# Who splits the first head's keys and queries, and how many idle transposes stand ahead of the first scores

## The reference

```python
q_bucket = sum((q @ proj > 0) * 2**arange(6));  k_bucket likewise
scores = where(q_bucket == k_bucket, q @ k.T / 8, -1e9)
attn = softmax(scores) @ v                       # x = heads side by side
x = sigmoid(causal_conv5(x, conv_w)) * (x @ w_val) @ w_out
xk, xr = mixes of x and the token before it (mu_k, mu_r)
out = sigmoid(xr @ w_r) * (relu(xk @ w_k)**2 @ w_v)
```

## Time and profile before

| | |
|---|---|
| median of 3 runs | 484.13 us (483.76 to 484.45) |
| the profiled execution | 483.76 us, span 482.0 us |
| TensorE matmuls busy | 471.7 us (98% of the span) |
| VectorE, ScalarE, GpSimd busy | 345.4, 279.0, 260.0 us |

### The profile page before, as it was taken

How to read it: one execution, slowest core, us unless ns; L and a number is a source line. 1 busy time by engine, 2 the same in 40 slices (tenths; PEclk the granted TensorE clock), 3 DMA queues, 4 the chain that set the end, 5 groups by cost and what they waited for, 6 DMA issues and landing times.

```text
span 482.0 us, 9492 instructions
## 1 busy us (share of the span) xinstructions
PE 471.7 (98%) x3541; PEld 400.3 (83%) x3541; DVE 345.4 (72%) x607; ACT 279.0 (58%) x597; POOL 260.0 (54%) x258
## 2 busy tenths in 40 slices
PE   7899999999999999999999999999999999999997
PEld 6766767666676776777779999999999999999997
DVE  5887897988888888887747977876668569326211
ACT  4977878878787987876745451442443353344230
POOL 5795647374472745652197683575455457346140
PEclk9999999999999999999999999999999999999999
DMA  6210310404021030200220001001000000100101
GB/s 231 67 55 18 106 48 4 136 17 137 16 62 78 18 136 18 71 19 18 88 87 1 3 1 45 0 1 46 2 1 29 17 2 1 45 1 1 45 1 44
DMA packets 10557, 20.69 MB, mean 43 GB/s; under 512 B 1680, under 2 KB 6928, under 8 KB 10512
## 3 DMA queue, kind: packets, MB, share of 16 engines
q1 hardware_dynamic: 10224, 19.94, 12.6%
q10 hardware_dynamic: 288, 0.15, 0.1%
HBM read 16.94 MB, written 3.15 MB: 42 GB/s over the span
## 4 chain that ended last, share of the span: by engine, by line
PE 74%; DVE 13%; issue 6%; ACT 3%; POOL 2%; DMA 2%; SPq 0%; DVEq 0%; ACTq 0%; POOLq 0%
PE ps L732 24%; PE ps L720 14%; PE ps L740 11%; PE ps L696 10%; PE ps L685 10%; DVE tmp_b L1011 2%; DVE gate L920 2%; ACT probs L497 2%; PE ps L706 2%; DVE tmp_b L986 1%; DVE tmp_a L988 1%; DVE negmax L877 1%; DVE pt L884 1%; PE ps L668 1%; DVE x L910 1%
## 5 line engine op out<-in xcount | busy, mean ns | idle before, releaser
L877 DVE TENSOR_REDUCE negmax<-ps 128x1 f32<-128x768 f32 x96 | 91.7, 956 | 23.6 <-PE ps L685 22.9
L685 PE MATMUL ps<-k,q 128*128 128x384 f32 x384 | 92.2, 362 | 3.4 <-ACT probs L497 2.8
L497 ACT ACTIVATE probs<-ps,negmax 128x768 f32<-128x768 f32 x96 | 86.5, 901 | 10.4 <-DVE negmax L877 10.0
L696 PE MATMUL ps<-ident,probs 128*128 128x128 f32 x576 | 82.3, 275 | 1.2
L696 PEld LDWEIGHTS ps<-ident,probs 128*128 128x128 f32 x576 | 66.8, 140 | 11.9 <-DVE pt L884 4.7
L685 PEld LDWEIGHTS ps<-k,q 128*128 128x128 f32 x384 | 62.8, 189 | 15.4 <-ACT probs L497 10.6
L720 PE MATMUL ps<-pt,vals 128*64 128x384 f32 x384 | 68.8, 494 | 0.0
L447 POOL TENSOR_TENSOR h_lo<-tmp_b,h_hi 128x256 fp32r<-128x256 f32 x48 | 39.3, 824 | 45.2 <-ACT h_hi L599 45.2
L505 ACT ACTIVATE pt<-ps 128x384 f32<-128x384 f32 x96 | 46.9, 488 | 18.8 <-PE ps L696 15.0
L732 PE MATMUL ps<-xk_hi,w_hi 128*128 128x256 f32 x192 | 53.9, 281 | 0.3 <-POOL xk_lo L441 0.3
L884 DVE COPY pt<-ps 128x384 f32<-128x384 f32 x96 | 52.1, 542 | 2.8 <-PE ps L696 2.8
(11 more groups left out here) (86 smaller groups left out, 1107.0 us busy)
## 6 DMA issues: line engine op xcount, KB each, us to landing
w_raw<-w SPq DMA_DIRECT2D x8, 640.0 KB, 6.1
raw_q<-qT SPq DMA_DIRECT2D x8, 384.0 KB, 4.5
raw_k<-kT SPq DMA_DIRECT2D x8, 384.0 KB, 3.4
vals<-v SPq DMA_DIRECT2D x16, 192.0 KB, 2.4
out<-w_raw SPq DMA_DIRECT2D x24, 128.0 KB, 1.7
w_raw<-w SPq DMA_DIRECT2D x4, 512.0 KB, 3.3
codes_b<-codes ACTq DMA_DIRECT2D x1, 128.0 KB, 4.3
proj_bd<-proj ACTq DMA_DIRECT2D x1, 16.0 KB, 3.4
```

Of the source, the lines that this page charges most:

```text
L497: act.activation(probs[par][:, :], score[par], ACT.Exp, bias=negmax[:, t:t + 1], accum_out=sums[:, t, 0:1]).then_inc(exp_done, 1)
L685: last = pe.matmul(ps[:, 2 * par + half, 0:HALF], qq[h][:, q], kk[h][:, half * HALF:(half + 1) * HALF], start=first, stop=not first)
L696: last = pe.transpose(tbank[u][:, k * P:(k + 1) * P], probs[g % 2][:, kt * P:(kt + 1) * P], ident[:, :])
L877: dve.tensor_reduce(negmax[:, t:t + 1], score[g % 2], AX.XY, ALU.max, negate=True).then_inc(max_done, 1)
```

## The change

GpSimd no longer makes the low keys of head 0: it starts with the low queries of head 0, then low keys and low queries of head 1. VectorE makes the low keys of head 0, in a new function `first_low_keys`, after the first of its two casts of head 0's high keys and ahead of `bits_out(0)`; the second cast of head 0 moves behind `bits_out(0)`. `high_keys` on VectorE now makes one half at a time, and the wait for the keys' load stands once ahead of the first. TensorE has 10 idle transposes ahead of `scores(0)` instead of 14.

```diff
--- before.py
+++ after.py
@@ -364,9 +364,9 @@
                                base=0, pattern=[[-1, P]], channel_multiplier=1).then_inc(ident_up, 1)
 
             pool.wait_ge(ident_up, 1)
-            for head in range(2):
-                low_keys(head)
-                low_queries(head)
+            low_queries(0)
+            low_keys(1)
+            low_queries(1)
             pool.wait_ge(qlo_done, 2)
 
             for i in range(PAIRS):
@@ -757,7 +757,7 @@
             pe.wait_ge(codes_in, 16)
             for j in range(4):
                 match(0, j)
-            keep_busy(14)
+            keep_busy(10)
             scores(0)
             scores(1)
             for g in range(PAIRS * TILES):
@@ -883,12 +883,12 @@
                 dve.wait_ge(tr_done[1], g + 1)
                 dve.tensor_copy(pt[head % 2][:, 3:6, tt * P:(tt + 1) * P], tbank3[1]).then_inc(up_done[1], 1)
 
-            def high_keys(head):
-
-                rows, n = (LO, HI)[head % 2], head % SETS
-                dve.wait_ge(k_in, 16)
-                for part in ((LO, HI), (HI, LO))[head % 2]:
-                    dve.tensor_copy(k2[n][part, :], raw_k[0][rows, :]).then_inc(khi_done, 1)
+            def high_keys(head, part):
+                dve.tensor_copy(k2[head][part, :], raw_k[0][(LO, HI)[head], :]).then_inc(khi_done, 1)
+
+            def first_low_keys():
+                dve.wait_ge(khi_done, 1)
+                dve.tensor_tensor(k1[0][HI, :], raw_k[0][LO, :], k2[0][LO, :], ALU.subtract).then_inc(klo_done, 1)
 
             def add_eps(head):
                 cols = slice(head % 2 * KT, head % 2 * KT + KT)
@@ -924,10 +924,14 @@
             dve.memset(sums[:, :, 1:2], 1e-9).then_inc(eps_up, 1)
             dve.memset(x[:, :, 0:HALO], 0.0).then_inc(halo_up, 1)
             scale_queries(0)
-            high_keys(0)
+            dve.wait_ge(k_in, 16)
+            high_keys(0, LO)
+            first_low_keys()
             bits_out(0)
+            high_keys(0, HI)
             hot_keys(0, A)
-            high_keys(1)
+            high_keys(1, HI)
+            high_keys(1, LO)
             tile_max(0)
             tile_max(1)
             hot_keys(0, B)
```

## The result

The changed kernel takes 484.87 us (median of 10 runs, 484.59 to 486.28), the kernel before beside it 483.93. The ratio is 1.0019, with a 95% interval of 1.0010 to 1.0027, so +0.94 us with some 0.4 us either way. The forecast was +1.01. One of the ten timings of the kernel before, 1178.58 us, lies far outside the others and is left out of the ratio. The profiled execution of the changed kernel has a span of 483.0 us, before 482.0.

A forecast was written before the change was run, and what follows sets the result against it. TensorE was taken as nearly always busy from 40 us, the start as set by VectorE; bits 1.73 us later less 0.72 gave +1.01 us on the 484.13 median, so 485.1 us, range 483.9 to 486.2.

The forecast's parts named there:

- The block on the new subtraction: VectorE's first low keys, blocked by GpSimd's low queries until 7.51, end 0.81 us later: 2.45 us instead of 0.95.
- Rival 2: VectorE's new subtraction is not blocked; first maximum at 10.42, -0.49 us, 483.6 us; chance 0.05.
- Rival 1: VectorE's subtraction gets in before GpSimd, head 0's second cast is blocked instead; +0.38 us, 484.5 us; chance 0.08.
- The hidden cast: Head 0's second key cast, behind `bits_out`, fits VectorE's 0.66 us wait for the matches; otherwise it would cost 0.59.
- the four transposes: TensorE's idle transposes before the first scores, ten for fourteen: worth nothing in the old order, 0.2 us in the new.
- The sum: Tile 0's first maximum at 11.92 against 10.91: bits 1.73 us later less 0.72, so +1.01 us.
- one piece of 0.71 us in it is a wait on GpSimd: VectorE's first cast of head 1 takes 1.27 us, its sisters 0.55 or 0.56, held by GpSimd's low queries.
- The 0.72: Saving from bits to first maximum, 3.73 us becoming 3.01, because head 1's cast is no longer blocked by GpSimd.
- Rival 3, the clock: TensorE's clock falls to half pace after idling 1.8 us before the matches; 2.3 us more, 487.4 us; chance 0.06.
- Rival 4, absorption: About half the shift is absorbed in TensorE's 5 us idle within the first 40 us; 484.6 us; chance 0.07.

The follow-up runs named there:

- run 1: Changed kernel with GpSimd's first low queries held until VectorE's new subtraction is done; ratio 1.0011 to the kernel before, first key cast to first maximum 6.27 us.
- run 2: Changed kernel with head 0's low queries replaced by a GpSimd zero fill that reads nothing; ratio 0.9988 to the kernel before.
- run 4: Changed kernel with 14 idle transposes again instead of 10; ratio 1.0028 to the kernel before, first key cast to first maximum 6.35 us.
- run 5: Kernel before with 10 idle transposes instead of 14 and nothing else; ratio 0.9999, first key cast to first maximum 5.64 us.
- run 8: Kernel before, unchanged, profiled once more in a single execution; first key cast to first maximum 5.63 us, no ratio of its own.
- run 9: Changed kernel, profiled once more in a single execution; first key cast to first maximum 6.65 us, no ratio of its own.
- run 7: Kernel before with head 1's casts after two maxima, its low queries before low keys, 10 transposes, head 0's second key cast on ScalarE; ratio 0.9995.
- run 11: The same kernel as run 7, timed again in five rounds; ratio 0.9991 to the kernel before, first key cast to first maximum 5.00 us.

## Why the prediction was right

*The block on the new subtraction* (2.45 us, tail of 0.81 for 768 columns) came out to the hundredth, in two profiles. Runs 1 and 2 show that it is a wait and what it waits for: 0.95 us if GpSimd comes later, 0.95 us if GpSimd only writes. Rival 2's world without blocking exists, but only without GpSimd's reads. Rival 1 (VectorE first) did not happen by itself; forced, in run 1, it costs +0.64 in distance, of which 0.26 is the semaphore's.

*The hidden cast* (8.80, in VectorE's wait for the matches) and *the four transposes* (10.77 for the first scores, their end ahead of the casts' 11.76) stood as worked out; the transposes' worth of 0.2 us is 0.21 in run 4, and their worth of nothing in the old order is run 5.

*The sum* was +1.73 - 0.72 = +1.01. The total is right, but the step "the start of the kernel is set by VectorE, and one piece of 0.71 us in it is a wait on GpSimd" is only half of it. The 0.72 is no fixed saving: it depends on how early the bits happened to be in that execution. Runs 5 and 8 show the wait as 0.00 and 0.35 us with the maximum unmoved. Better put: before, GpSimd's two subtractions end 4.59 us after the first key cast, and 1.04 later comes the maximum; after, with keys that land before GpSimd asks, the bits end at 3.63, behind the blocked subtraction, and 3.01 later comes the maximum. 6.64 less 5.63 is the +1.01, and TensorE's pace at the start enters neither: run 9 has the slow projection (0.85 us a matmul) and the same distance, 6.65.

That the measured +0.94 is so near is in part luck, for its interval is some 0.4 us wide to either side. The forecast put +1.01 on the edge of what a measurement can tell from no change, which it took as 0.97 us; +0.94 falls just below that, while the interval of 1.0010 to 1.0027 leaves no change out.

*Rival 3, the clock.* The 2.11 us that TensorE idled ahead of the matches did no harm: matches take 0.81 and the eight matmuls of scores 1.63 us, no slower than before. *Rival 4, absorption*, did not come about: the first maximum stands 0.87 us later, head 2's scores 0.88, and the span is 1.0 longer. From the first maximum to the end it is 471.1 us before and 471.2 after; where the difference arises is open.

What the forecast had no term for is the arrival of the keys. In runs 1 and 4 the first cast of the keys, which waits for their load, starts at 6.14 and 6.22 us, in the other eleven profiles at 5.07 to 5.52. Keys that land after GpSimd has begun turn the collision round, as in run 4. There the changed order would cost about 0.5 us and not 1.0 (an estimate: 6.35 of run 4, less 0.21 for the four transposes, less 5.63, if the kernel before keeps its 5.63 then, which no profile shows). That the order of arrival was the one that the forecast assumed is thus a matter of the execution. How often the keys come late in timed runs isn't known; the gap between +0.94 and +1.01 is smaller than the noise and needs no cause.

## What to carry to other kernels

Work that is handed from GpSimd to VectorE to run beside it can end up behind it. In these runs a cast or a two-input subtraction of VectorE and a subtraction of GpSimd took nearly the sum of their durations, whoever came second: in the changed kernel the pair took 2.48 us, from the end of the cast ahead of it (5.69) to 8.17, where the two alone take 1.81 and 0.95. What did run beside a subtraction of another engine without growing longer was a fill on GpSimd (run 2), the hot keys on VectorE, which come from PSUM and took their 1.14 us beside GpSimd, and the copy that runs 7 and 11 hand to ScalarE:

```profile
6.03 0.83 ACT L539 ACTIVATE k<-raw_k 64x768 fp32r<-64x768 f32 x1
```

It took 0.83 us beside GpSimd's subtraction of 6.08, where a like copy takes 0.84 with GpSimd idle. Look for instructions that are longer than their sisters: here such waits counted as busy time and appeared in no list of waits. Before counting a removed wait as a gain, ask whether it is slack that other executions have filled already: profile the same kernel twice, and take as the bound what doesn't move.

## What the runs showed of the hardware that was not expected

TensorE's pace doubles at a time that differs between executions, with the same instructions ahead of it. In the changed kernel's profile it doubled inside the first 18 idle transposes (3.66 us in all, have 4.10): up to the fifteenth they start 0.21 us apart, the last ones 0.11. In run 5 the projection still ran at the low pace, 0.85 us a matmul:

```profile
1.53 4.10 PE L750 MATMUL ps<-ident 128*128 128x128 f32 x18 [1.53 <-POOL ident L363]
...
6.21 0.85 PE L659 MATMUL ps<-raw_q,proj_bd 128*32 128x384 f32 x1
```

against 0.48 in the changed kernel:

```profile
5.57 0.48 PE L659 MATMUL ps<-raw_q,proj_bd 128*32 128x384 f32 x1
```

The granted clock reads 1.00 in all of these stretches, so here the paces of like instructions tell the level (2.4 or 1.2 GHz) and the column doesn't. The doubling inside the transposes also bears on the sentence of the Trainium skill named under rival 3 ("TensorE: Matmul & The Clock Gate", Part 4), that transposes do not count as busy: nothing but transposes had run by then. So either they count in this kernel, or the pace doubled without any counted work; no run here tells the two apart.
